# Linear attention, experts and a max MLP on one core: sums and floors moved to GpSimd, rows turned by transposes

## The chip, the core and the metric

The kernel runs on one core of a Trainium2 chip. A core has five engines with a queue each: TensorE (PE, matmuls into the PSUM banks; its weight loads are listed apart as PEld), VectorE (DVE), ScalarE (ACT), GpSimd (POOL) and SyncE (SP, which here only issues DMAs). They wait for each other through semaphores. The metric is the device time of one execution in microseconds, lower is better.

## The reference

```python
def _attn_ref(r, k, v, w, u):                     # B, H, S, D = 4, 8, 768, 48
    state = np.zeros((B, H, D, D))
    for t in range(S):
        cur = np.einsum('bhd,bhe->bhde', u[None] * kt, vt)
        y[:, :, t] = np.einsum('bhd,bhde->bhe', rt, state + cur)
        state = wt[:, :, :, None] * state + np.einsum('bhd,bhe->bhde', kt, vt)

def reference(...):
    x = attn_out.transpose(0, 2, 1, 3).reshape(3072, 384)
    x = _moe_ref(x, expert_emb, tau, w1, w2)      # one of 8 experts per token, by the largest
                                                  # dot with the unit embeddings, over tau
    h = max(x @ m1, x @ m2, x @ m3); return h @ w_out
```

What is computed in the part that the change touches: for each batch and head the gated linear attention, whose term r.(u*k) for a token's own key stands apart; the turning of its output into rows of tokens in DRAM; and for each token the dots with the 8 expert embeddings, their largest and the first expert that has it.

## The kernel before

**Stages.** Attention fills the first 176 us, the routing table lies between 176 and 198 us, and then the experts in slots of 432 tokens and the max MLP in blocks of 512 run on PE to the end. The change lies in the first stage alone.

**Pairs.** Attention goes over n = 0 to 15, a pair of heads of one batch each (four pairs to a batch, PAIRS = 4). The 768 positions of a pair are 6 chunks of 128 (CH); a half h is 3 chunks (HALF). The order on each engine is written out by hand as a loop over n, and only semaphores tie the engines together. For pair n+1, in the loop body of n:

- PE: rows_of(n-1, 0), keys(n) (turns the scaled keys to rows), turn_raw(n+1, "k"), scores(n, 1), turn_raw(n+2, "w"), rows_of(n-1, 1), turn_raw(n+1, "r"), key_values(n), mix_values(n) for both halves, mix_state(n), scores(n+1, 0). turn_raw turns the inputs from positions to columns by transposes, and the turn of w waits until VectorE has read the same banks for the keys.
- VectorE: mask(n, 0), own_of(n+1), keys_of(n+1), mask(n, 1), prefix_of(n+1), carry(n), receptance_of(n+1), suffix_of(n+2). suffix_of and prefix_of are the running products of the decay w, from behind and from the front, as scans of 774 elements (L948, L959). prefix_of first takes the floor of the chunks' products (L957) and its reciprocal (L958). own_of sums the products r*k*u of each position (L991). mask places the scores above the diagonal (L999).
- GpSimd: own_products(n+2) and own_times_u(n+2) make r*k and r*k*u in rku (L567, L572), and own_diagonal(n+1) spreads the own sums on a diagonal in score (L589), on which the mask of pair n+1 waits. Before own_products it waits for suffix_ok, before own_diagonal for prefix_ok, so each begins when a scan has ended.
- ScalarE: copies out of PSUM, among them x_cols (L695), x_rows (L703) and dot_parts (L705), and the stores of token rows to DRAM.

**Rows.** rows_of(n, h) multiplies the attention output x_cols (columns by positions) from the right by to_rows, 104 wide: an arranged identity of 96 columns that turns the pair into rows and puts its heads in order, and 8 columns of the expert embeddings, which give the pair's part of the dots. An fp32 matmul is two instructions in the trace, a transpose is one; so a half is x6.

**Batches.** When four pairs are done, add_dots(b) sums their four parts of the dots (L1021) and largest_of(b) finds the largest per token (L1028, L1029), in the body n = 4, 8 and 12, between carry and receptance; first_of(b) finds the first expert (L1035 to L1038) at the same place in n = 5, 9 and 13. The last batch follows behind the loop.

## Time and profile before

| | |
|---|---|
| median of 3 runs | 740.96 us (740.53 to 742.77) |
| profiled execution | 742.08 us, its span 740.3 |
| granted TensorE clock, mean | 0.98 |
| PE busy | 696.4 us, 94% of the span |
| VectorE busy | 415.2 us, 56% |
| ScalarE busy | 278.1 us, 38% |
| GpSimd busy | 129.3 us, 17% |

The profile is one execution. Shares over the span mix the stages: VectorE's share is 9 tenths or more in the slices up to about 150 us and falls behind them, while PE's is 9 tenths nearly throughout. In a timeline row the first number is the start, the second the time from the first start to the last end of what is merged there (x6: six instructions); a bracket tells how long the engine was idle before it and what ended that. Successive instructions of VectorE overlap by some 0.08 us, and a PE group's end is modelled, so the distance between starts tells more than the durations do.

### The profile page before, as it was taken

The page shows a single profiled execution, that of the slowest core. Times are in us where ns is not written, and L with a number is a line of the kernel's source. Part 1 is how long each engine was busy: PE and PEld are TensorE (multiplying, and loading weights), DVE is VectorE, ACT ScalarE, POOL GpSimd, SP SyncE. Part 2 cuts the span into 40 slices and gives each one's busy share as a digit, 9 for nine tenths or more (in the row PEclk, how much of TensorE's full clock was granted, in tenths as well). Part 3 has the DMA queues.
Part 4 walks back from the last instruction along what each step waited for, and adds up shares of the span by engine and source line. Part 5 has one row for each costly group of instructions (what it writes and reads, how often), then busy time and mean ns, then how long its engine had stood idle before and what let it go on. Part 6 is the DMA issues. An engine that isn't in the chain of part 4 may idle for free.

```text
span 740.3 us, 12783 instructions
## 1 busy us (share of the span) xinstructions
PE 696.4 (94%) x4794; PEld 626.3 (85%) x4794; DVE 415.2 (56%) x611; ACT 278.1 (38%) x584; POOL 129.3 (17%) x120
## 2 busy tenths in 40 slices
PE   6899999984799999999999999999999999999995
PEld 6788788873799999999999988888988988989875
DVE  7899999995766666554554545324233243242331
ACT  3355555555366665454444443112022021120110
POOL 4644444430522210000000000010100200201102
PEclk9999999998799999999999999999999999999998
DMA  9999998911475754433433400010000100100001
GB/s 147 171 193 190 143 161 144 221 34 34 144 230 168 212 170 128 130 119 93 127 107 105 127 21 1 1 43 1 22 22 1 43 0 1 43 1 21 23 0 43
DMA packets 148679, 66.44 MB, mean 90 GB/s; under 512 B 119560, under 2 KB 146320, under 8 KB 148624
## 3 DMA queue, kind: packets, MB, share of 16 engines
q1 hardware_dynamic: 131024, 51.13, 32.3%
q0 software_dynamic: 3072, 9.54, 4.1%
q10 hardware_dynamic: 14528, 5.03, 3.1%
q8 instruction: 35, 0.57, 0.3%
q14 instruction: 20, 0.16, 0.1%
HBM read 56.14 MB, written 9.54 MB: 89 GB/s over the span
## 4 chain that ended last, share of the span: by engine, by line
PE 85%; DVE 5%; issue 3%; SPq 2%; POOL 2%; DMA 1%; ACT 0%; DVEq 0%; POOLq 0%
PE bank L1375 13%; PE bank L1377 13%; PE bank L1376 13%; PE score_banks L1375 7%; PE score_banks L1377 7%; PE score_banks L1376 7%; PE turn_banks L1375 3%; PE turn_banks L1377 3%; PE turn_banks L1376 3%; PE bank L1493 3%; PE bank L1464 2%; PE score_banks L1422 2%; PE turn_banks L1409 2%; PE bank L1480 2%; DVE key_s L973 2%
## 5 line engine op out<-in xcount | busy, mean ns | idle before, releaser
L641 POOL DMA_INDIRECT out_dram<-o_put,slot_tok x24 | 25.2, 1052 | 438.8 <-DVE o_put L1345 438.8
L1375 PE MATMUL bank<-hh,w2h 128*128 128x432 f32 x192 | 69.0, 359 | 0.0
L1377 PE MATMUL bank<-hh,w2l 128*128 128x432 f32 x192 | 68.8, 358 | 0.0
L1376 PE MATMUL bank<-hl,w2h 128*128 128x432 f32 x192 | 68.8, 358 | 0.0
L1296 DVE SCALAR_TENSOR_TENSOR hl<-score_banks,hh 128x432 fp32r<-128x432 f32 x48 | 29.2, 608 | 66.6 <-ACT hh L841 65.7
L892 ACT CAST gh<-g 128x512 fp32r<-128x512 f32 x36 | 22.4, 621 | 106.7 <-PE bank L1377 60.7
L1375 PE MATMUL score_banks<-xh,w1h 128*128 128x432 f32 x144 | 53.6, 372 | 0.5 <-DVE xl L1256 0.5
L841 ACT ACTIVATE hh<-score_banks 128x432 fp32r<-128x432 f32 x48 | 25.5, 531 | 73.3 <-PE score_banks L1377 73.3
L1376 PE MATMUL score_banks<-xl,w1h 128*128 128x432 f32 x144 | 52.2, 363 | 0.0
L1377 PE MATMUL score_banks<-xh,w1l 128*128 128x432 f32 x144 | 52.2, 362 | 0.0
L1375 PE MATMUL bank<-moh,gh 128*128 128x384 f32 x144 | 48.8, 339 | 0.9 <-DVE gl L1363 0.9
L1354 DVE TENSOR_TENSOR g<-bank,g 128x512 f32<-128x512 f32 x18 | 12.5, 692 | 66.0 <-ACT g L888 66.0
L1376 PE MATMUL bank<-mol,gh 128*128 128x384 f32 x144 | 48.7, 338 | 0.0
L1377 PE MATMUL bank<-moh,gl 128*128 128x384 f32 x144 | 48.7, 338 | 0.0
L1345 DVE TENSOR_SCALAR o_put<-bank,slot_gate 128x384 f32<-128x384 f32 x24 | 14.8, 618 | 52.8 <-PE bank L1377 52.8
L1354 DVE TENSOR_TENSOR g<-turn_banks,g 128x512 f32<-128x512 f32 x18 | 12.5, 692 | 56.7 <-ACT g L888 56.7
L1375 PE MATMUL score_banks<-bh,mh 128*128 128x512 f32 x108 | 42.5, 394 | 0.0
L1375 PE MATMUL turn_banks<-bh,mh 128*128 128x512 f32 x108 | 42.5, 394 | 0.0
L1375 PE MATMUL bank<-bh,mh 128*128 128x512 f32 x108 | 42.5, 394 | 0.0
L1377 PE MATMUL turn_banks<-bh,ml 128*128 128x512 f32 x108 | 42.3, 392 | 0.0
L1377 PE MATMUL score_banks<-bh,ml 128*128 128x512 f32 x108 | 42.3, 392 | 0.0
L1377 PE MATMUL bank<-bh,ml 128*128 128x512 f32 x108 | 42.3, 392 | 0.0
(221 smaller groups left out, 1734.0 us busy)
## 6 DMA issues: line engine op xcount, KB each, us to landing
w_raw<-in_moe_w_dram SPq DMA_DIRECT2D x77, 384.0 KB, 3.3
raw_w<-in_w_dram SPq DMA_DIRECT2D x32, 144.0 KB, 3.9
raw_r<-in_r_dram SPq DMA_DIRECT2D x32, 144.0 KB, 4.6
vals<-in_v_dram SPq DMA_DIRECT2D x32, 144.0 KB, 3.6
x_tokens<-x_rows ACTq DMA_DIRECT2D x32, 144.0 KB, 3.5
raw_k<-in_k_dram SPq DMA_DIRECT2D x30, 144.0 KB, 4.4
w_raw<-in_moe_w_out_dram SPq DMA_DIRECT2D x3, 384.0 KB, 3.2
w_more<-in_moe_w_dram SPq DMA_DIRECT2D x2, 384.0 KB, 5.4
```

What stands on the lines that cost most here:

```text
L641: pool.indirect_dma_start(out=out, out_offset=bass.IndirectOffsetOnAxis(ap=slot_tok[:, n:n + 1], axis=0), in_=o_put[:, n % SB, :], in_offs ...
L841: act.activation(hh[:, f % UPS, :], bank[2 + f % 3][:, 0:SLOT], ACT.Relu).then_inc(hh_ok, 1)
L892: act.copy(gh[:, f, :], g2[:, :]).then_inc(gh_ok, 1)
L973: dve.tensor_tensor(key_s[:, n % 2].rearrange("q (x c) t -> q x c t", x=2), turned_half(turn_banks), products[:, n % 2, 0, :, 1:P + 1].rea ...
L1296: dve.scalar_tensor_tensor(out=hl[:, f % UPS, :], in0=bank[2 + f % 3][:, 0:SLOT], scalar=0.0, in1=f32(hh[:, f % UPS, :]), op0=ALU.max, op1 ...
L1354: dve.tensor_tensor(g1[:, :], bank[3 * (f % 2) + 1][:, :], g0[:, :], ALU.max).then_inc(g1_ok, 1)
L1375: pe.matmul(dst, sh, mh_, start=first, stop=False)
L1376: pe.matmul(dst, sh, ml_, start=False, stop=False)
L1377: return pe.matmul(dst, sl_, mh_, start=False, stop=last)
L1409: ins = pe.transpose(bank[x + (2 if name == "r" else 0)][:, j * P:(j + 1) * P], src, ident[:, :])
L1422: ins = pe.matmul(bank[2 + i][:, c * P:(c + 1) * P], key_s[rows, n % 2, HALF * h + c], rec_s[rows, n % 2, HALF * h + c], start=True, stop= ...
L1493: ins = pe.matmul(bank[7][:, c * (PW + E):(c + 1) * (PW + E)], x_cols[:, h, c], to_rows[:, h, p, :], start=True, stop=True)
```

## The change

Three things change in the attention stage.

- GpSimd gets more to do. own_times_u adds, after the multiplication by u, the upper 24 columns of each group of 48 in rku to the lower 24; VectorE's own_of reduces 24 columns. first_prefixes(n) takes the floor of the chunks' products into fore_floor; VectorE waits for it (fore_ok) and takes the reciprocal from there. dots_of(b) sums the four parts of a batch's dots in two steps, behind own_diagonal in the bodies n = 4, 8 and 12.
- On VectorE largest_of(b) stands behind receptance_of in n = 5, 9, 13 and first_of(b) behind it in n = 6, 10, 14.
- rows_of makes three transposes by the identity and then three matmuls of x_cols with emb_cols (8 columns). The heads' order, which to_rows gave for the second half, is now made by ScalarE's copy out of the bank (a negative step over the two 64-wide parts). The four copies that filled to_rows go.

```diff
             def own_times_u(n):
                 p = n % PAIRS
-                four = rku[:, n % 2].rearrange("q (c h) d -> q c h d", h=2)
-                pool.tensor_tensor(out=four, in0=four,
-                                   in1=u_row[...].broadcast_to([P, CH, 2, D]),
-                                   op=ALU.mult).then_inc(own_prod, 1)
+                both = rku[:, n % 2].rearrange("q (c h) d -> q c h d", h=2)
+                after(pool.tensor_tensor(out=both, in0=both,
+                                         in1=u_row[...].broadcast_to([P, CH, 2, D]),
+                                         op=ALU.mult))
+                pool.tensor_tensor(out=rku[:, n % 2, :, 0:D // 2], in0=rku[:, n % 2, :, 0:D // 2],
+                                   in1=rku[:, n % 2, :, D // 2:], op=ALU.add).then_inc(own_prod, 1)
...
+            def first_prefixes(n):
+                pool.wait_ge(suffix_ok, n + 1)
+                if n:
+                    pool.wait_ge(prefix_ok, n)
+                pool.tensor_scalar(fore_floor[:, :], products[:, n % 2, 0, :, 0], 1 / (LIMIT * 1e4), None, ALU.max
+                                   ).then_inc(fore_ok, 1)
...
+            def dots_of(b):
+                rows = slice(CH * b, CH * (b + 1))
+                pool.wait_ge(x_ready, 2 * PAIRS * (b + 1))
+                after(pool.tensor_tensor(out=two_parts[:, :, :, :], in0=dot_parts[:, rows, 0:2, :],
+                                         in1=dot_parts[:, rows, 2:4, :], op=ALU.add))
+                pool.tensor_tensor(out=dots[:, rows, :], in0=two_parts[:, :, 0, :], in1=two_parts[:, :, 1, :],
+                                   op=ALU.add).then_inc(dots_ok, 1)
...
+            first_prefixes(0)
             pool.wait_ge(prefix_ok, 1)
             own_products(0)
-            pool.wait_ge(suffix_ok, 2)
+            first_prefixes(1)
             own_times_u(0)
...
             for n in range(ALL - 1):
+                if n:
+                    first_prefixes(n + 1)
                 if n + 2 < ALL:
-                    pool.wait_ge(suffix_ok, n + 2)
                     own_products(n + 2)
                     own_times_u(n + 2)
                 pool.wait_ge(prefix_ok, n + 2)
                 own_diagonal(n + 1)
+                if n and n % PAIRS == 0:
+                    dots_of(n // PAIRS - 1)
...
             def prefix_of(n):
                 dve.wait_ge(suffix_ok, n + 1)
-                if n:
-                    dve.wait_ge(prefix_ok, n)
-                after(dve.tensor_scalar(fore_set[:, :, 0], products[:, n % 2, 0, :, 0], 1 / (LIMIT * 1e4), None, ALU.max))
-                after(dve.reciprocal(fore_set[:, :, 0], fore_set[:, :, 0]))
+                dve.wait_ge(fore_ok, n + 1)
+                after(dve.reciprocal(fore_set[:, :, 0], fore_floor[:, :]))
...
-                dve.tensor_reduce(out=own[...], in_=rku[:, n % 2], axis=AX, op=ALU.add)
+                dve.tensor_reduce(out=own[...], in_=rku[:, n % 2, :, 0:D // 2], axis=AX, op=ALU.add)
...
                 carry(n)
-                if n > 1 and n % PAIRS == 0:
-                    add_dots(n // PAIRS - 1)
-                    largest_of(n // PAIRS - 1, after)
-                if n > PAIRS and n % PAIRS == 1:
-                    first_of(n // PAIRS - 1, after)
                 if n + 1 < ALL:
                     receptance_of(n + 1)
-                else:
+                if n > PAIRS and n % PAIRS == 1:
+                    largest_of(n // PAIRS - 1, after)
+                if n > PAIRS and n % PAIRS == 2:
+                    first_of(n // PAIRS - 1, after)
+                if n + 1 == ALL:
                     judge()
...
                 for c in range(HALF):
-                    ins = pe.matmul(bank[7][:, c * (PW + E):(c + 1) * (PW + E)], x_cols[:, h, c],
-                                    to_rows[:, h, p, :], start=True, stop=True)
+                    pe.transpose(bank[7][:, c * P:(c + 1) * P], x_cols[:, h, c], ident[:, :])
+                for c in range(HALF):
+                    at = HALF * P + c * E
+                    ins = pe.matmul(bank[7][:, at:at + E], x_cols[:, h, c], emb_cols[:, h, p, :], start=True, stop=True)
```

PE's order before, for one pair: from scores(n, 1) (L1422) over the turn of w (L1409, into turn_banks), rows_of, the turn of r, key values (L1442), mix_values (L1464) and mix_state (L1480) to the next scores.

```order
L1422 MATMUL score_banks<-rec_s,key_s 128x128 x6
L1409 MATMUL turn_banks<-ident,raw_w 128x128 x6
L1493 MATMUL bank<-to_rows,x_cols 128x104 x3
L1409 MATMUL score_banks<-ident,raw_r 128x128 x6
L1442 MATMUL bank<-vals,key_rows 64x48 x10
L1464 MATMUL bank<-score,vals 64x128 x12
L1480 MATMUL bank<-rec_s,state 64x128 x10
L1422 MATMUL score_banks<-rec_s,key_s 128x128 x6
```

The same place after the change; the lines of before L1422, L1409, L1442, L1464 and L1480 are now L1440, L1427, L1460, L1482 and L1498.

```order
L1440 MATMUL score_banks<-rec_s,key_s 128x128 x6
L1427 MATMUL turn_banks<-ident,raw_w 128x128 x6
L1511 MATMUL bank<-ident,x_cols 128x128 x3
L1514 MATMUL bank<-emb_cols,x_cols 128x8 x3
L1427 MATMUL score_banks<-ident,raw_r 128x128 x6
L1460 MATMUL bank<-vals,key_rows 64x48 x10
L1482 MATMUL bank<-score,vals 64x128 x12
L1498 MATMUL bank<-rec_s,state 64x128 x10
L1440 MATMUL score_banks<-rec_s,key_s 128x128 x6
```

The order of the steps is the same; each rows_of is two groups in place of one, and here a matmul of the source counts as one.

VectorE before, at the batch steps of body n = 4: the prefix scan (L959), carry (L1006, L1015), the batch's sum and largest, receptance (L983), the suffix scan (L948).

```order
L959 SCALAR_TENSOR_TENSOR products<-decay,fore_set 128x774
L1006 SCALAR_TENSOR_TENSOR bank<-total,bank 128x240
L1015 TENSOR_TENSOR state<-bank,products 128x5x48
L1021 TENSOR_REDUCE dots<-dot_parts 128x48
L1028 TENSOR_REDUCE best<-dots 128x6
L1029 TENSOR_TENSOR maxed<-dots,best 128x48
L983 TENSOR_TENSOR rec_s<-score_banks,products 128x768
L948 SCALAR_TENSOR_TENSOR products<-decay,back_set 128x774
```

VectorE after, in body n = 5, from the second mask (L1018) on.

```order
L1018 COPY_PREDICATED score<-later,score_banks 128x2x3x128
L977 RECIPROCAL fore_set<-fore_floor 128x6
L978 SCALAR_TENSOR_TENSOR products<-decay,fore_set 128x774
L1025 SCALAR_TENSOR_TENSOR bank<-total,bank 128x240
L1034 TENSOR_TENSOR state<-bank,products 128x5x48
L1002 TENSOR_TENSOR rec_s<-score_banks,products 128x768
L1047 TENSOR_REDUCE best<-dots 128x6
L1048 TENSOR_TENSOR maxed<-dots,best 128x48
L969 SCALAR_TENSOR_TENSOR products<-decay,back_set 128x774
```

The sum is gone from VectorE, the largest stands behind receptance, and the floor ahead of the reciprocal is gone.

GpSimd after, in bodies n = 4 and 5: products, times u, half-add, diagonal, the batch's two sums, the next floor.

```order
L578 TENSOR_TENSOR rku<-raw_r,raw_k 128x576
L583 TENSOR_TENSOR rku<-rku,u_row 128x576
L586 TENSOR_TENSOR rku<-rku 128x12x24
L602 AFFINE_SELECT score<-own 128x1536
L611 TENSOR_TENSOR two_parts<-dot_parts 128x96
L613 TENSOR_TENSOR dots<-two_parts 128x48
L569 TENSOR_SCALAR fore_floor<-products 128x6
```

Before, only the first, second and fourth of these kinds stood here (L567, L572, L589).

## Rows read from the trace of the kernel before

**Rows 1.** Windows between starts of scores(n, 0): range, length, busy us (count) by engine, clock, DMA.
```profile
39.49:48.66 9.17, 8.84 (x124) 7.85 (x124) 9.05 (x12) 5.39 (x14) 4.39 (x3) 1.00 1.19 184
...
57.83:68.00 10.17, 8.85 (x125) 7.85 (x124) 9.94 (x15) 6.44 (x16) 4.38 (x3) 1.00 1.15 190
68.00:78.28 10.28, 8.86 (x124) 7.86 (x124) 10.09 (x15) 5.55 (x14) 4.39 (x3) 1.00 0.90 146
```

**Rows 2.** Timeline, VectorE, pair 3's period: start us, us, engine, line, op, shapes, [idle before].
```profile
51.09 0.74 DVE L991 TENSOR_REDUCE own<-rku 128x12 f32<-128x576 f32 x1
...
51.74 0.95 DVE L973 TENSOR_TENSOR key_s<-turn_banks,products 128x768 f32<-128x768 f32 x1
...
53.55 0.15 DVE L957 TENSOR_SCALAR fore_set<-products 128x6 f32<-128x6 f32 x1
...
53.96 1.77 DVE L959 TENSOR_TENSOR_SCAN products<-decay,fore_set 128x774 f32<-128x774 f32 x1
...
55.76 0.66 DVE L1006 TENSOR_TENSOR_SCAN bank<-total,bank 128x240 f32<-128x240 f32 x1
...
56.78 0.95 DVE L983 TENSOR_TENSOR rec_s<-score_banks,products 128x768 f32<-128x768 f32 x1
...
57.64 1.76 DVE L948 TENSOR_TENSOR_SCAN products<-decay,back_set 128x774 f32<-128x774 f32 x1
```

**Rows 3.** Timeline, PE, the same period and the next scores and rows.
```profile
50.82 0.82 PE L1409 MATMUL turn_banks<-ident,raw_k 128*128 128x128 f32 x6
...
52.84 0.85 PE L1409 MATMUL turn_banks<-ident,raw_w 128*128 128x128 f32 x6 [0.33 <-DVE key_s L973]
...
53.52 0.81 PE L1493 MATMUL bank<-to_rows,x_cols 128*128 128x104 f32 x6
...
54.17 0.82 PE L1409 MATMUL score_banks<-ident,raw_r 128*128 128x128 f32 x6
...
54.92 0.79 PE L1442 MATMUL bank<-vals,key_rows 128*64 128x48 f32 x20
...
57.83 0.94 PE L1422 MATMUL score_banks<-rec_s,key_s 64*128 64x128 f32 x12
...
58.70 0.92 PE L1493 MATMUL bank<-to_rows,x_cols 128*128 128x104 f32 x6
```

**Rows 4.** PE's weight loads: timeline of L1531; groups by line, mean ns behind the busy us.
```profile
173.90 0.30 PEld L1531 LDWEIGHTS turn_banks<-bad,all_ones 128*128 128x128 f32 x2
...
L1493 PEld LDWEIGHTS bank<-to_rows,x_cols 128*128 128x128 f32 x144 | 17.9, 191 | 1.4
...
L1409 PEld LDWEIGHTS turn_banks<-ident,raw_k 128*128 128x128 f32 x72 | 8.2, 141 | 0.0
```

**Rows 5.** Timeline, batch steps: VectorE's sum and first-expert product, GpSimd's select beside it.
```profile
65.95 0.48 DVE L1021 TENSOR_REDUCE dots<-dot_parts 128x48 f32<-128x192 f32 x1
...
76.12 0.64 DVE L1035 TENSOR_TENSOR maxed<-maxed,expert_no 128x48 f32<-128x48 f32 x1
...
75.16 1.55 POOL L589 TENSOR_SCALAR_AFFINE_SELECT score<-own 128x1536 f32<-128x1536 f32 x1 [2.58 <-DVE products L959]
```

**Rows 6.** Timeline, pairs 0 to 2: GpSimd, then VectorE.
```profile
24.72 1.75 POOL L567 TENSOR_TENSOR rku<-raw_r,raw_k 128x576 f32<-128x576 f32 x1 [2.50 <-DMA raw_r<-in_r_dram]
26.54 1.41 POOL L572 TENSOR_TENSOR rku<-rku,u_row 128x576 f32<-128x576 f32 x1
...
22.25 0.75 DVE L991 TENSOR_REDUCE own<-rku 128x12 f32<-128x576 f32 x1 [1.41 <-POOL rku L572]
...
27.02 2.55 DVE L948 TENSOR_TENSOR_SCAN products<-decay,back_set 128x774 f32<-128x774 f32 x1
31.02 1.01 DVE L999 COPY_PREDICATED score<-later,score_banks 128x768 f32<-128x768 int32 x1 [1.45 <-POOL score L589]
```

**Rows 7.** Timeline, ScalarE: the copy of the turned embeddings.
```profile
8.65 0.44 ACT L733 COPY to_rows<-bank 48x64 f32<-48x64 f32 x2 [0.78 <-PE bank L1392]
```

**Rows 8.** Timeline, PE: the key values of pair 15.
```profile
169.93 0.79 PE L1442 MATMUL bank<-vals,key_rows 128*64 128x48 f32 x20 [1.01 <-issue]
```

More of the change, by code:

```diff
@@ L133, in linear_attention_moe_max_mlp @@
     x_rows = sb("x_rows", [P, XR, HALF, PW])
-    to_rows = sb("to_rows", [P, 2, PAIRS, PW + E])
+    emb_cols = sb("emb_cols", [P, 2, PAIRS, E])
     squares = sb("squares", [E, DM])
@@ L701, in tokens_of @@
                     act.wait_ge(x_stored[s % XR], 16 * (s // XR))
-                src = bank[7][:, 0:HALF * (PW + E)].rearrange("q (c e) -> q c e", c=HALF)
-                act.copy(x_rows[:, s % XR], src[:, :, 0:PW]).then_inc(rows_out, 1)
+                src = bank[7][:, 0:HALF * P].rearrange("q (c i d) -> q c i d", c=HALF, i=2)[:, :, ::1 - 2 * h, 0:D]
+                act.copy(x_rows[:, s % XR].rearrange("q c (i d) -> q c i d", i=2), src).then_inc(rows_out, 1)
                 first = CH * b + HALF * h
-                act.copy(dot_parts[:, first:first + HALF, p, :], src[:, :, PW:]).then_inc(x_ready, 1)
+                act.copy(dot_parts[:, first:first + HALF, p, :],
+                         bank[7][:, HALF * P:HALF * (P + E)].rearrange("q (c e) -> q c e", c=HALF)).then_inc(x_ready, 1)
                 act.wait_ge(rows_out, s + 1)
@@ L724, in _ @@
             act.wait_ge(rows_clear, 1)
-            for x in range(2):
-                for i in range(2):
-                    rows = slice(64 * (i ^ x), 64 * (i ^ x) + D)
-                    act.copy(to_rows[rows, x, :, D * i:D * (i + 1)],
-                             ident[rows, rows].unsqueeze(1).broadcast_to([D, PAIRS, D])).then_inc(emb_ready, 1)
             act.wait_ge(emb_turned, 1)
@@ L732, in _ @@
                 rows = slice(64 * i, 64 * i + D)
-                act.copy(to_rows[rows, :, :, PW:], bank[7][rows, 0:2 * PAIRS * E].rearrange(
+                act.copy(emb_cols[rows, :, :, :], bank[7][rows, 0:2 * PAIRS * E].rearrange(
                     "q (x p e) -> q x p e", x=2, p=PAIRS)).then_inc(emb_ready, 1)
@@ L990, in own_of @@
                     dve.wait_ge(own_ready, n - 1)
-                dve.tensor_reduce(out=own[:, n % 2].rearrange("q c h -> q (c h)"), in_=rku[:, n % 2], axis=AX, op=ALU.add
+                dve.tensor_reduce(out=own[:, n % 2].rearrange("q c h -> q (c h)"), in_=rku[:, n % 2, :, 0:D // 2], axis=AX, op=ALU.add
                                   ).then_inc(own_sum, 1)
```

11 lines of the change are left out of this document (7 added, 4 removed).

## Prediction, made before the changed kernel was run

> **What bounds the kernel now.** I read the page's busy shares first: PE 94% of the span. But every edit lies in the first 176 us, the attention stage, so I cut that stage at the starts of scores(n, 0), the PE step that opens the work on head pair n. From 39.49 us on, the distance is 9.17 us; in six of the next twelve it is 10.17 or 10.28 [rows 1]. In 9.17 us VectorE is busy 9.05 and PE 8.84: two engines sit at the limit together.
>
> The chain of waits says the same of one period. VectorE's starts follow each other without a gap: own sum 51.09, keys 51.74, floor 53.55, prefix scan 53.96, carry 55.76, receptance 56.78, suffix scan 57.64 [rows 2]. PE looks as if it had 0.33 us of air, its wait for keys at 52.84, but that wait is a detour of its own path: the turn of k ends at 50.82 + 0.82 = 51.64, VectorE's keys runs from 51.74 to 52.69 and the turn of w follows at 52.84; of these 1.2 us PE can fill 0.87 with scores(n, 1), as long as scores(n, 0) takes from 57.83 to 58.70 [rows 2, 3]. From the key values at 54.92 the route through carry (55.76), state and receptance (56.78 + 0.95 = 57.73) reaches scores at 57.83, and PE's own steps end there too [rows 2, 3]. So what is added on PE anywhere in a period lengthens it; what is taken from VectorE alone does not shorten it. **The six long periods are VectorE's**: batch sums and largest values in one, the first-expert step in the next, 1.00 and 1.11 us more; PE waits in them.
>
> **What the change takes from VectorE.** Per period the floor goes: its 0.15 us and the handover to the reciprocal, 0.18. The own sum reduces 24 instead of 48 columns per group; from 0.74 us for 576 elements I put 288 at 0.45, 0.29 less (0 to 0.37). Three batch sums of 0.48 go [rows 5]. The largest and the first steps stay but stand behind receptance, off PE's path, half a us or so each. VectorE's work per period falls to 8.7, and to 9.2 or 9.35 where a batch step stands. Three times two long periods therefore lose what made them long: 3 x 2.11 = 6.3 us, the whole gain. The rest of VectorE's saving is idle time, because PE is at 9.17.
>
> **What it adds to PE.** A half of rows_of was 3 fp32 matmuls, 6 in the trace, each with its own 128-column load; the half at 53.52 ends at 54.17, 0.108 us for each [rows 3]. It becomes 3 transposes and 3 matmuls with 8 moving columns, in the trace 3 + 6 = 9. What does one of 8 columns cost? The nearest row has a single moving column: the 128x1 matmul of L1531. Its two weight loads together take 0.30 us and one such load takes 0.19, so the second began 0.11 after the first [rows 4]: the load sets the pace, however few columns move. By plain count a half gains 3 x 0.107 = 0.32 us. Two things take some off: a transpose's load is 0.05 shorter than a matmul's (141 against 191 ns) [rows 4], which shows at the first load of the half at 58.70, and the last matmul streams 8 columns, not 104, ahead of the next group (0.04). I take +0.24 for the half at 58.70 and +0.28 for that at 53.52, +0.52 a period (bounds 0.45 to 0.64). As receptance and keys have slack now, 0.02 may come back: 9.67 us.
>
> The Trainium skill has a rule that would make the new form cheap: the page "TensorE: Matmul & The Clock Gate", section Back-to-back issue gap, gives 1 to 64 moving columns an issue floor of about 25 ns. By it the six small matmuls are an estimated 0.15 us, and the half would get shorter. L1531's loads speak against it; the rule is given for a matmul alone.
>
> Twelve periods from 39.49: before 6 x 9.17 + 3 x 10.17 + 3 x 10.28 = 116.4; after 12 x 9.67 = 116.0, plus what follows.
>
> **What it adds to GpSimd.** Per pair: a floor on 6 columns, which I put at 0.2 (0.1 to 0.4; VectorE took 0.15), and a half-add of 288 elements. The multiplication by u takes 1.41 for 576 [rows 6]; 0.8 for the half (0.7, in proportion, to 1.41, no saving). In the loop GpSimd has room, it is busy 4.39 of 9.17 us [rows 1], but not at any moment: a VectorE scan and a GpSimd instruction exclude each other. The suffix scan at 27.02 took 2.55 us instead of 1.76 because GpSimd's product at 26.54 ran until 27.95 [rows 6], and the small product on VectorE at 76.12 took 0.64, until the select begun at 75.16 had ended [rows 5]. The Trainium skill, page "GPSIMD Engine Reference", the table's line on SBUF interfaces, names this contention for VectorE instructions with two SBUF inputs or in a 2-port mode; both rows fit it, and whether the reciprocal is held no row here shows.
>
> Counted from scores(n, 0): the suffix scan ends near 1.6, floor 1.7, products 1.9 to 3.3, times u to 4.8, half-add 4.85 to 5.65. The prefix scan wants to begin at 5.3, so it waits 0.3 and ends at 7.4. Carry must wait for the key values until 7.5: the stall is covered by 0.1 us. In the two periods behind a largest or a first step GpSimd's chain is 0.5 to 0.7 later, the half-add begins just when the scan wants to and lies wholly in front of it or between, and carry comes 0.2 to 0.4 late. That is 0.6 a batch, for two batches 1.2 us (0 to 2.5); the third falls on pair 14, where PE turns no w and has air. The batch sums on GpSimd (about 0.7) lie before the suffix scan and cost 0.1.
>
> **What moves at no cost.** ScalarE's four copies into to_rows go; the next thing it does, the copy of the turned embeddings, waited 0.78 us for PE behind them anyway [rows 7]. Its copy out of the rows bank reads the same 288 elements in another order. SP's store of a batch's dots waits for GpSimd instead of VectorE, a period later at most; SP has by then no load to issue that a pair waits for behind it, since the stores stand behind all raw loads. VectorE's reciprocal waits for GpSimd's floor, 3 us old by then. If GpSimd were late, keys and masks would not be queued behind that wait, but the prefix scan and carry would.
>
> **The first two pairs.** Here VectorE waits for GpSimd: 1.41 us at the own sum of 22.25, 1.45 at the mask of 31.02 [rows 6]. Two half-adds and a floor with their gaps delay the own sum to about 24.3. The prefix scan behind it now meets the products of pair 2, which start at 24.72 in both kernels since they wait for raw_r, and comes 2.7 us or more late. Some of it is absorbed by the old waits at 31.02 and by loads that have come meanwhile. Followed on to scores(2, 0) it leaves 39.49 + 1.4 us (0 to 3).
>
> **The end.** Pair 14: +0.2. Pair 15 has three halves in line: one ahead of ScalarE's copies on which the key values of 169.93 wait [rows 8], then its own two: +0.8.
>
> **Sum**, against the profiled run's 742.08 us (span 740.3 and 1.8 around it): start +1.4, twelve periods -0.4, collisions +1.2, pair 14 +0.2, end +0.8 gives +3.2; I round down to +3.0 for the front of pair 2, where much waits on loads. Behind 176 us nothing changes. The median of the runs shown, 740.96, is 1.1 below the profiled run; the same difference gives 744.0.
>
> **Rivals.**
> (a) The small matmuls' loads hide behind their neighbours and only columns count: 8 of 104 columns' 0.108 is 0.01 each, with some issue up to 0.025. A half is then 3 x 0.108 + 6 x 0.01 to 0.025 = 0.38 to 0.47, about 0.23 shorter, and PE's period 8.7. The Trainium skill's issue floor above points the same way. Now VectorE sets it: 8.7 and a scan held 0.5 behind GpSimd, 9.2, and 0.48 or 0.67 more in the batch steps' periods, of which I let 2.9 us show in all. 12 x 9.2 + 2.9 = 113.3 against 116.4, start +1.4, end -0.7: -2.4, or 738.6, faster; with GpSimd's adds at their low bound 736. For it: nothing but the columns; against it: [rows 4]. It decides from about 0.075 us for a small matmul down: a half then costs 3 x 0.108 + 6 x 0.075 = 0.77, 0.12 more than now, 2 x 0.12 x 12 + 0.4 = 3.3 in all, and the 6.3 us won at the batch steps outweigh that, the start and the collisions together.
> (b) GpSimd's half-add is 1.2 us or more, or the floor 0.4: the prefix scan ends past 7.5 in every period, and 0.25 x 12 + 1.5 in the start and the collisions are added: 748.5. For it: only 0.1 us covers it.
> (c) The old rows pace was partly slack and half of the 0.52 is absorbed: 12 x 0.26 = 3.1 less, 740.9, no change. For it: PE's 0.33 wait; against it: that wait is a round trip of PE's own.
>
> **Chances.** Forecast 0.60, at 744.0 (own range 742 to 746.5, from the bounds 0.45 to 0.64 and those of the collisions); (a) 0.15, half of it below 738.7; (b) 0.13; (c) 0.12. About 0.3%, 2.2 us, is what a measurement of this kernel can tell from no change: below 738.7 faster, above 743.2 slower. The forecast case has 0.17 of its 0.60 below 743.2. Slower 0.43 + 0.13 = 0.56; same 0.17 + 0.12 + 0.07 = 0.36; faster 0.08. The range for 8 in 10: 739.5 to 748.0, which leaves out the low end of (a) and the top of (b).
>
> **What would show it.** Right: periods near 9.7, none at 10.2 but two or four near 9.9 to 10; PE's rows half 0.9 us or more with loads 0.11 apart; VectorE idle about 0.6 a period; the prefix scan at 2.0 us rather than 1.77; scores(2, 0) near 40.9. Wrong: loads of the small matmuls closer than 0.075 apart; periods below 9.4; a prefix scan that isn't lengthened. A clock below 1.0 between 40 and 170 us would upset all of it.

## Result and profile after the change

| | before | after |
|---|---|---|
| median of 5 runs each | 740.96 us (739.6 to 742.94) | 746.71 us (744.27 to 747.55) |
| ratio | | 1.0052, 95% interval 1.0029 to 1.0075 |
| profiled execution, its span | 742.08, 740.3 us | 746.71, 744.9 us |
| granted TensorE clock, mean | 0.98 | 0.976 |
| PE busy | 696.4 us | 707.0 us |
| VectorE busy | 415.2 us | 406.2 us |
| GpSimd busy | 129.3 us | 153.2 us |

The kernel became slower by 0.3 to 0.75%. VectorE lost 9 us of work, PE gained 10.6 and GpSimd 24. The difference of the two profiled spans, 4.6 us, lies in these stretches:

| stretch | before | after | difference |
|---|---|---|---|
| to scores(2, 0) | 39.49 | 41.92 | +2.43 |
| the twelve periods from there to scores(14, 0) | 116.37 | 117.04 | +0.67 |
| pair 14 | 9.03 | 9.05 | +0.02 |
| scores(15, 0) to the last batch sum | 11.37 | 11.98 | +0.61 |
| from that sum to the end | 564.1 | 564.9 | +0.8 |

The last line is mostly scatter. Nothing is changed there, and in the eleven other profiles of this study with the same work behind the sum it lies between 562.2 and 564.7 us.

Windows of after between starts of scores(n, 0) (range, length, then busy us and count of PE, weight loads, VectorE, ScalarE and GpSimd, granted clock, DMA share, GB/s):

```profile
41.92:51.65 9.73, 9.40 (x131) 8.40 (x130) 8.76 (x11) 5.46 (x14) 5.37 (x5) 1.00 0.73 154
61.38:71.11 9.73, 9.40 (x132) 8.41 (x130) 8.77 (x11) 5.45 (x14) 6.02 (x7) 1.00 0.74 154
90.56:100.44 9.88, 9.46 (x131) 8.39 (x130) 9.12 (x14) 5.44 (x14) 6.78 (x5) 1.00 0.72 151
```

Against [rows 1]: every period is 9.73 us, with the batch sums in it (second line) or without; only the two behind a first-expert step are 9.88. PE's work rose from 8.84 to 9.40 us, the same 0.56 by which the period rose. VectorE's fell from 9.05 to 8.76 and bought nothing.

Timeline of after, PE, in the period from 61.38 (start us, us, engine, line, op, shapes, [idle before and what ended it]), to be laid beside [rows 3]:

```profile
62.25 0.55 PE L1511 MATMUL bank<-ident,x_cols 128*128 128x128 f32 x3
62.63 0.73 PE L1514 MATMUL bank<-emb_cols,x_cols 128*128 128x8 f32 x6
63.22 0.74 PE L1450 MATMUL bank<-ident,key_s 128*128 128x128 f32 x5
63.80 0.82 PE L1427 MATMUL turn_banks<-ident,raw_k 128*128 128x128 f32 x6
...
65.82 0.84 PE L1427 MATMUL turn_banks<-ident,raw_w 128*128 128x128 f32 x6 [0.33 <-DVE key_s L992]
66.50 0.49 PE L1511 MATMUL bank<-ident,x_cols 128*128 128x128 f32 x3
66.83 0.73 PE L1514 MATMUL bank<-emb_cols,x_cols 128*128 128x8 f32 x6
67.42 0.85 PE L1427 MATMUL score_banks<-ident,raw_r 128*128 128x128 f32 x6
68.20 0.79 PE L1460 MATMUL bank<-vals,key_rows 128*64 128x48 f32 x20
68.82 1.50 PE L1482 MATMUL bank<-score,vals 128*64 128x128 f32 x24
```

The second half of rows runs from 66.50 to 67.42: 0.92 us for 3 turns and 6 instructions of 8 columns, where the old one took 0.65 from 53.52 to 54.17. The six small ones alone take 0.59, 0.10 each. The first half takes 0.97. PE's wait for the keys is 0.33 as before.

VectorE and GpSimd in the same period, beside [rows 2]:

```profile
63.77 0.43 DVE L1010 TENSOR_REDUCE own<-rku 128x12 f32<-128x288 f32 x1
64.71 0.96 DVE L992 TENSOR_TENSOR key_s<-turn_banks,products 128x768 f32<-128x768 f32 x1 [0.51 <-issue]
...
66.72 1.93 DVE L978 TENSOR_TENSOR_SCAN products<-decay,fore_set 128x774 f32<-128x774 f32 x1
69.03 0.66 DVE L1025 TENSOR_TENSOR_SCAN bank<-total,bank 128x240 f32<-128x240 f32 x1 [0.39 <-PE bank L1460]
```

```profile
63.04 0.23 POOL L569 TENSOR_SCALAR fore_floor<-products 128x6 f32<-128x6 f32 x1 [2.50 <-DVE products L969]
63.23 1.42 POOL L578 TENSOR_TENSOR rku<-raw_r,raw_k 128x576 f32<-128x576 f32 x1
64.73 1.41 POOL L583 TENSOR_TENSOR rku<-rku,u_row 128x576 f32<-128x576 f32 x1
66.22 0.80 POOL L586 TENSOR_TENSOR rku<-rku 128x288 f32<-128x288 f32 x1
```

The half-add ends at 67.02, and the prefix scan begun at 66.72 takes 1.93 instead of 1.77: the scan is held until the half-add is done. It does no harm here, since carry then waits 0.39 us for PE. VectorE's idle time is 0.9 us a period.

### The profile page after: what moved, and what is told of

Read it like the earlier page. It is cut to its first block, busy times and chain, and to the rows that moved or that the text cites. A ratio compares the mean times of both kernels' runs of the same rounds, so it can differ in the third digit from the quotient of the medians.

```text
span 744.9 us, 12991 instructions
## 1 busy us (share of the span) xinstructions
PE 707.0 (95%) x4890; PEld 636.2 (85%) x4890; DVE 406.2 (55%) x592; ACT 277.4 (37%) x580; POOL 153.2 (21%) x158
## 3 DMA queue, kind: packets, MB, share of 16 engines
q0 software_dynamic: 3072, 9.54, 4.0%
HBM read 56.14 MB, written 9.54 MB: 88 GB/s over the span
## 4 chain that ended last, share of the span: by engine, by line
PE 88%; DVE 5%; issue 3%; POOL 2%; DMA 1%; ACT 0%; ACTq 0%; DVEq 0%; POOLq 0%
PE bank L1393 13%; PE bank L1395 13%; PE bank L1394 13%; PE score_banks L1393 7%; PE score_banks L1395 7%; PE score_banks L1394 7%; PE turn_banks L1393 3%; PE turn_banks L1395 3%; PE turn_banks L1394 3%; PE bank L1482 3%; PE bank L1514 2%; PE score_banks L1440 2%; PE turn_banks L1427 2%; PE bank L1511 2%; PE bank L1498 2%
```

## The experiments

"Period" is the distance between starts of scores(n, 0) without batch steps; b1 and b2 are the two long ones behind a batch. "Pair 1" and "pair 2" are the starts of their scores.

| kernel | median us | ratio, interval | pair 1 | pair 2 | period | b1, b2 | last sum |
|---|---|---|---|---|---|---|---|
| before | 740.96 | | 28.13 | 39.49 | 9.17 | 10.17, 10.28 | 176.25 |
| after | 746.71 | 1.0052, 1.0029 to 1.0075 | 29.38 | 41.92 | 9.73 | 9.73, 9.88 | 179.99 |
| e1 rows alone | 748.35 | 1.0103, 1.0077 to 1.0129 | 27.34 | 39.19 | 9.73 | 10.72, 10.53 | 182.58 |
| e2 all but rows | 738.82 | 0.9955, 0.9937 to 0.9974 | 29.64 | 40.42 | 9.23 | 9.37, 9.58 | 172.75 |
| e3 batch steps alone | 737.10 | 0.9941, 0.9919 to 0.9962 | 28.24 | 38.55 | 9.17 | 9.66, 9.88 | 171.85 |
| e4 after, clock kept up | 742.73 | 1.0009, 0.9994 to 1.0023 | 29.89 | 39.62 | 9.73 | 9.73, 9.88 | 177.69 |
| e5 e3 + floor | 737.03 | 0.9926, 0.9908 to 0.9944 | 27.82 | 36.99 | 9.17 | 9.66, 9.88 | 170.23 |
| e6 e3 + half-add | 741.69 | 0.9986, 0.9974 to 0.9998 | 29.58 | 40.35 | 9.47 | 9.57, 9.79 | 175.63 |
| e7 e5, clock kept up | 736.38 | 0.9910, 0.9892 to 0.9928 | 28.54 | 37.71 | 9.17 | 9.66, 9.88 | 170.93 |
| e9 before again | 743.03 | 1.0003, 0.9985 to 1.0021 | 28.20 | 40.44 | 9.17 | 10.17, 10.27 | 177.22 |
| e10 e6, half-add later | 741.72 | 0.9981, 0.9970 to 0.9993 | 30.20 | 39.74 | 9.35 | 9.89, 10.10 | 175.30 |
| e11 e5, steps spread | 736.19 | 0.9907, 0.9891 to 0.9922 | 27.92 | 37.09 | 9.17 | 9.37 to 9.53 | 169.55 |
| e12 e11, clock kept up | 734.88 | 0.9891, 0.9875 to 0.9906 | 28.20 | 37.37 | 9.17 | 9.36 to 9.52 | 169.83 |

### The three parts of the change

**e1** is the kernel before with the new rows alone:

```diff
-                    ins = pe.matmul(bank[7][:, c * (PW + E):(c + 1) * (PW + E)], x_cols[:, h, c],
-                                    to_rows[:, h, p, :], start=True, stop=True)
+                    pe.transpose(bank[7][:, c * P:(c + 1) * P], x_cols[:, h, c], ident[:, :])
+                for c in range(HALF):
+                    at = HALF * P + c * E
+                    ins = pe.matmul(bank[7][:, at:at + E], x_cols[:, h, c], emb_cols[:, h, p, :], start=True, stop=True)
```

> The kernel before with nothing changed but the turning of rows (three transposes and three 8-column matmuls, ScalarE's reordering copy). Theory (PE's weight loads are added to every period): the normal period is 9.73 us as in the changed kernel, not 9.17, while the six batch-step periods stay VectorE's at 10.2 and 10.3, so 6 x 0.56 = 3.4 us in the twelve periods and 0.6 at the end, +4 us, ratio 1.005 to 1.006. Rival (PE had slack, the collisions with GpSimd made the changed kernel slower): normal period 9.2 to 9.4, +1 us or less.

Its windows:

```profile
39.19:48.92 9.73, 9.40 (x131) 8.41 (x131) 9.11 (x12) 5.41 (x14) 4.38 (x3) 1.00 1.19 184
58.65:69.37 10.72, 9.40 (x130) 8.39 (x131) 10.02 (x15) 6.45 (x16) 4.38 (x3) 1.00 1.07 171
```

The period is that of after to the hundredth, so the new rows alone set it: +0.56. The long periods were a miss, and with them the ratio: the last sum is 6.3 us later than before, not 4. PE's new work did not vanish in VectorE's long periods, it was added to them: in full in the first of a batch (10.72), by 0.25 in the second (10.53), where the first-expert product now takes 0.34 instead of 0.64 [rows 5], as GpSimd's select beside it is nearer to its end. The batch steps stood between carry and receptance, where PE waits, and the rows stand where VectorE waits. Both are pieces of one path, and their prices add up.

**e2** is the change with the old rows (the same lines turned back, with to_rows and its copies).

> The changed kernel with the old turning of rows: all that moved to GpSimd, and the batch steps behind receptance. Theory: PE's 9.17 us is the floor of the period, VectorE needs 8.7 and is held about 0.4 by the half-add, so normal periods are 9.2 to 9.3 and batch-step periods at most 9.8: twelve periods 112.5 instead of 116.4, -3 to -4 us with a start that costs up to 1, ratio 0.995. Rival (GpSimd's adds are what made the changed kernel slower): periods of 9.7 remain and the ratio is 1.000 to 1.005.

Without the rows the rest of the change is a gain of 0.3 to 0.6%, with the periods that were expected. **e3** takes from that rest the batch steps alone: the sums on GpSimd, largest and first behind receptance.

```diff
+                if n and n % PAIRS == 0:
+                    dots_of(n // PAIRS - 1)
...
-                if n > 1 and n % PAIRS == 0:
-                    add_dots(n // PAIRS - 1)
-                    largest_of(n // PAIRS - 1, after)
-                if n > PAIRS and n % PAIRS == 1:
-                    first_of(n // PAIRS - 1, after)
                 if n + 1 < ALL:
                     receptance_of(n + 1)
...
+                if n > PAIRS and n % PAIRS == 1:
+                    largest_of(n // PAIRS - 1, after)
+                if n > PAIRS and n % PAIRS == 2:
+                    first_of(n // PAIRS - 1, after)
```

> The kernel before with only the batch's sum of dots on GpSimd and largest and first steps behind receptance one period later; floor, own sum and rows as before. Theory (the whole gain lies in the batch steps): normal periods stay 9.17, batch-step periods fall from 10.17 and 10.28 to about 9.66 and 9.85, for VectorE still has to do them, 3 x 0.95 = -2.8 us, some of it lost to the sum on GpSimd that lies beside the suffix scan (up to 3 x 0.5). -1.5 to -2.8 us, ratio 0.997. Rival (PE's path hides them wholly once they are behind receptance): -6 us.

The batch steps alone bring as much as all of e2, whose interval overlaps. The periods came as expected, the gain was larger: 4.4 us at the last sum instead of at most 2.8. The first two batches give 1.8, the third, whose steps fall mostly behind the twelve periods, 1.7, and pair 2 is 0.9 earlier, of which the last section tells. **e5** adds the floor on GpSimd, **e6** in its place the half-add, with the floor left on VectorE:

```diff
+                pool.tensor_tensor(out=rku[:, n % 2, :, 0:D // 2], in0=rku[:, n % 2, :, 0:D // 2],
+                                   in1=rku[:, n % 2, :, D // 2:], op=ALU.add).then_inc(own_prod, 1)
...
-                dve.tensor_reduce(out=own[:, n % 2].rearrange("q c h -> q (c h)"), in_=rku[:, n % 2], axis=AX, op=ALU.add
+                dve.tensor_reduce(out=own[:, n % 2].rearrange("q c h -> q (c h)"), in_=rku[:, n % 2, :, 0:D // 2], axis=AX, op=ALU.add
```

> The batch-steps-only kernel plus the floor on GpSimd; own sum and rows as before. Theory (normal periods are PE's 9.17, batch-step periods VectorE's sum): VectorE is 0.18 shorter, so normal periods stay 9.17, and the two long periods of a batch fall from 9.66 and 9.88 to about 9.5 and 9.7; -0.9 us against the batch-steps-only kernel, ratio 0.993. Rival (the floor's 0.23 us on GpSimd pushes products and times u into the prefix scan): periods 9.3 and no gain, ratio 0.995 or more.

> The batch-steps-only kernel plus the half-add on GpSimd and the shorter own sum; floor and rows as before. Theory (the half-add is what holds the prefix scan and lengthens the first pairs): VectorE is 0.3 shorter but is held about as long, so normal periods are 9.17 to 9.25, batch-step periods about 9.4 to 9.6, and scores(2, 0) comes 1 to 2 us later than in the batch-steps-only kernel: ratio 0.995, worse than batch steps alone by 0.5 to 1.5 us. Rival (the floor is what costs, the half-add is a gain): ratio below 0.993.

The floor's move costs nothing (e5 and e3 overlap), but it did not shorten the long periods as expected: they stay at 9.66 and 9.88, and e11 below shows why. The half-add takes back 0.45%: period 9.47, where 9.17 to 9.25 was expected, pair 1 at 29.58. Timeline of e6, VectorE:

```profile
52.22 0.44 DVE L1005 TENSOR_REDUCE own<-rku 128x12 f32<-128x288 f32 x1
52.90 0.96 DVE L987 TENSOR_TENSOR key_s<-turn_banks,products 128x768 f32<-128x768 f32 x1 [0.24 <-issue]
...
54.68 0.61 DVE L971 TENSOR_SCALAR fore_set<-products 128x6 f32<-128x6 f32 x1
55.33 0.19 DVE L972 RECIPROCAL fore_set<-fore_set 128x6 f32<-128x6 f32 x1
55.55 1.77 DVE L973 TENSOR_TENSOR_SCAN products<-decay,fore_set 128x774 f32<-128x774 f32 x1
```

And GpSimd beside it:

```profile
54.47 0.80 POOL L577 TENSOR_TENSOR rku<-rku 128x288 f32<-128x288 f32 x1
```

The half-add runs from 54.47 to 55.27. VectorE's floor of 6 elements, 0.15 us alone, begins at 54.68 and ends when the half-add does. The 0.3 us that the shorter own sum saves turn into a wait of 0.24 ahead of the keys (the view has it as issue; PE's turn of k ends just before), while the 0.45 lost behind them lie on the path, and 0.30 of it reaches the period.

In e2 the floor is on GpSimd, and the half-add of the same length holds the scan itself. VectorE, then GpSimd:

```profile
54.75 2.18 DVE L982 TENSOR_TENSOR_SCAN products<-decay,fore_set 128x774 f32<-128x774 f32 x1
```

```profile
54.51 0.79 POOL L586 TENSOR_TENSOR rku<-rku 128x288 f32<-128x288 f32 x1
```

The scan is 0.41 longer, but it began 0.22 earlier, as the floor isn't in front of it: period 9.23. So the floor's move is worth something only where the half-add has come as well.

**e10** is e6 with one more GpSimd instruction of 6 elements ahead of each pair's products, which puts the half-add later:

```diff
+                pool.tensor_scalar(delay_out[:, :], products[:, n % 2, 0, :, 0], 1 / (LIMIT * 1e4), None, ALU.max
+                                   ).then_inc(delayed, 1)
```

> The version with the half-add on GpSimd and the floor on VectorE (741.69 us, periods of 9.47 to 9.55 us), with one more GpSimd instruction of 6 elements ahead of the products of each pair, whose output nobody reads. It puts the half-add about 0.25 us later. My theory, that the half-add hurts there because it starts just ahead of VectorE's floor and holds it and the prefix scan behind: now floor and scan come first, the half-add is the one that waits, and the period falls to 9.2 to 9.35 us, the time to about 738.5 us, ratio 0.996. Rival, that the half-add costs by its length wherever it lies, or that GpSimd's chain is itself the late one: the period stays at 9.5 us or grows to 9.7 us, and the ratio is 0.999 to 1.002.

VectorE, then GpSimd:

```profile
53.96 0.15 DVE L982 TENSOR_SCALAR fore_set<-products 128x6 f32<-128x6 f32 x1
54.14 0.20 DVE L983 RECIPROCAL fore_set<-fore_set 128x6 f32<-128x6 f32 x1
54.37 2.10 DVE L984 TENSOR_TENSOR_SCAN products<-decay,fore_set 128x774 f32<-128x774 f32 x1
```

```profile
54.05 0.80 POOL L586 TENSOR_TENSOR rku<-rku 128x288 f32<-128x288 f32 x1
```

Half a hit. The half-add now begins 0.09 behind the floor's start, the floor takes 0.15 again and the period falls by 0.12, though the half-add still comes ahead of the scan and holds it for 0.3. That more GpSimd work makes the period shorter rules out the rival for the normal periods. The time did not follow: it is that of e6, not 738.5, for b1 and b2 grew by 0.3 each. In them the multiplication by u, made later by the extra instruction, reaches into VectorE's floor. GpSimd, then VectorE, in b1:

```profile
81.19 1.42 POOL L583 TENSOR_TENSOR rku<-rku,u_row 128x576 f32<-128x576 f32 x1
```

```profile
82.24 0.40 DVE L982 TENSOR_SCALAR fore_set<-products 128x6 f32<-128x6 f32 x1
```

In e6 the same floor takes 0.16, and the scan behind it 2.13; here the floor takes 0.40 and the scan 2.21. In these periods the rival's second half is right: GpSimd's chain is the late one.

### What a small matmul costs

**e8** is the change with one small matmul a half instead of three, 24 columns wide; it leaves out the dots of two chunks of three, so that tokens go to other experts and the part behind 176 us differs (761.33 us, not to be compared). Only the periods count.

```diff
-                for c in range(HALF):
-                    at = HALF * P + c * E
-                    ins = pe.matmul(bank[7][:, at:at + E], x_cols[:, h, c], emb_cols[:, h, p, :], start=True, stop=True)
+                ins = pe.matmul(bank[7][:, HALF * P:HALF * (P + E)], x_cols[:, h, 0],
+                                emb_cols[:, h, p, :].unsqueeze(1).broadcast_to([P, HALF, E]), start=True, stop=True)
```

> The changed kernel with one small matmul per half in place of three: it multiplies the first chunk by the embeddings three times over (24 moving columns), so the dots of two chunks in three are left out; four of the six small instructions go, the moving columns stay 24. Theory (each small instruction costs its 128-column load, 0.107 us): a half is 0.43 shorter, PE's period would be 8.87, and the period becomes what VectorE and GpSimd give in the kernel with the old rows, 9.2 to 9.3, batch-step periods 9.4 to 9.6; ratio 0.995 to 0.997. Rival (columns or the change between forms set the price): periods stay at 9.6 to 9.73 and the ratio at 1.005.

```profile
71.68 0.49 PE L1511 MATMUL bank<-ident,x_cols 128*128 128x128 f32 x3
72.00 0.30 PE L1512 MATMUL bank<-emb_cols,x_cols 128*128 128x24 f32 x2
72.15 0.85 PE L1427 MATMUL score_banks<-ident,raw_r 128*128 128x128 f32 x6
```

The half takes 0.47 instead of 0.92: four instructions less are 0.45 less, 0.11 each, with the same 24 columns in all. Instructions are paid here, each with its 128-column load, and columns are not. An instruction without such a load does not cost that much: the key values above, 20 instructions of 48 columns with loads of 64, run from 68.20 to 68.82, 0.03 each. Few columns behind a shorter load were not tried. The periods are 9.21 to 9.25 us, 9.44 behind a first-expert step: this is the world of rival (a), which had put them at 9.2. The expectation of the ratio was missed, for the reason above.

Behind each batch sum e8 has a period of 8.82 us. VectorE's scan in the period before it, and in it:

```profile
62.66 2.38 DVE L978 TENSOR_TENSOR_SCAN products<-decay,fore_set 128x774 f32<-128x774 f32 x1
71.90 1.77 DVE L978 TENSOR_TENSOR_SCAN products<-decay,fore_set 128x774 f32<-128x774 f32 x1
```

GpSimd's half-add in the same two:

```profile
62.62 0.80 POOL L586 TENSOR_TENSOR rku<-rku 128x288 f32<-128x288 f32 x1
71.93 2.33 POOL L586 TENSOR_TENSOR rku<-rku 128x288 f32<-128x288 f32 x1
```

In the first the half-add begins 0.04 ahead of the scan and holds it. In the second the scan gets in 0.03 ahead, and now the half-add is the one that waits (2.33 us) and nobody waits for it. A shift of 0.07 us between the two engines is the difference between 9.24 and 8.82, in all three batches. This shows what e10 aimed at; and 8.82 is PE's own period, for which 8.87 was expected.

### The start and the clock

**e4** is the change with 36 and 42 small bf16 matmuls on PE in the waits of pair 0, written to a bank that is not in use:

```diff
             def mix_state(n):
+                if n == 0:
+                    warm(42)
                 pe.wait_ge(state_ready, n + 1)
...
                 scores(n, 1)
+                if n == 0:
+                    warm(36)
```

> The changed kernel with 36 and 42 small bf16 matmuls on PE (without use) where PE waits in pair 0, ahead of the turn of w for pair 2 and ahead of the state product. Theory (the start's extra time is PE at half clock from 29 to 36 us behind its waits): granted clock stays 1.0 from 25 to 37 us, scores(1, 1) and the steps around it go at full pace, and scores(2, 0) starts at 39.5 instead of 41.9: 2.4 us less than the changed kernel, ratio to before 1.002 to 1.003. Rival (GpSimd's longer chain delays the start): scores(2, 0) stays at 41 to 42 and the ratio at 1.005.

A window of after, then of e4:

```profile
30.00:35.00 5.00, 5.00 (x30) 4.67 (x27) 2.37 (x3) 1.73 (x6) 3.62 (x4) 0.50 1.09 218
```

```profile
30.00:35.00 5.00, 4.67 (x50) 4.22 (x51) 4.67 (x5) 2.29 (x8) 3.13 (x5) 1.00 0.94 189
```

In after PE waits 2.57 us for VectorE's state at 25.9 to 28.47, and from 29.5 to 36.3 it runs at a granted clock of 0.50, the lower of the two levels: the turn of k takes 1.42 us to the next start instead of 0.75. Pair 1's period is 12.54 there and 9.73 in e4, though e4 was 0.51 later at pair 1. The clock is 2.8 us of the start in this profile; at the last sum e4 is 2.3 ahead, and its ratio is back at 1.

The wait alone does not bring this on. e8 and e10, which have no extra matmuls, wait 2.44 and 2.15 us at the same place and stay at 1.00 from there to 45 us, with 8.86 and 9.54 us for pair 1's period; e2 and e6 wait 3.7 us and have 0.50 for some 3.3 us, with 10.8. So how much of the 2.8 comes with the change and how much with the one execution stays open. A part of it is there in each run: the mean granted clock is 0.974 to 0.979 in the five of after and 0.978 to 0.987 in the twelve of e4.

**e7** puts 24 and 30 of them into e5.

> The batch-and-floor kernel with 24 and 30 small bf16 matmuls without use where PE waits in pair 0. Theory (a low-clock stretch in the first 40 us costs what a gap on PE brings on): granted clock 1.0 from 20 to 37 us and scores(2, 0) 1 us or more earlier than without them, about 37.5; ratio 0.991. Rival (the start waits for GpSimd and loads, whatever the clock): scores(2, 0) within 0.3 us of the batch-and-floor kernel's.

It settles nothing: e5 had the full clock from 20 us on without them, and pair 2 is no earlier (37.71 against 36.99).

**e9** is the kernel before, once more.

> The kernel before, unchanged, profiled and timed once more, to see how much of the start is the execution's own and not the kernel's. My theory: ratio 1.000 within 0.003; the periods behind pair 2 are 9.17 us again, those with batch steps 10.1 to 10.3 us, and the scores of pair 2 begin within 1 us of 39.5 us. Rival, that the 2.4 us by which the change was late at pair 2 are scatter of the first loads' landing: the scores of pair 2 begin here more than 1.5 us away from 39.5 us.

Pair 2 is at 40.44, 0.95 later than in the first profile, and the ratio is 1 within its interval. The first loads are not the reason. At pair 1 the two profiles are 0.07 apart and at pair 2's turn of w 0.19 (33.68 and 33.87); then e9 has a granted clock of 0.50 from 34.6 to 38.0, where the first profile has 1.00 throughout:

```profile
35.00:40.00 5.00, 5.00 (x71) 4.50 (x72) 4.18 (x6) 2.41 (x5) 2.14 (x2) 0.70 1.30 191
```

So the kernel before has such stretches too, in some executions, and of the +2.43 at pair 2 some 1 us may be the execution's own. Pair 1 is steadier. In the six profiles with a half-add (after, e2, e4, e6, e8, e10) it lies at 29.4 to 30.4, in the eight without one at 27.3 to 28.5: 29.9 on average against 28.1, so the half-add costs some 1.8 us there, whatever else is changed; e6 and e3, which differ by it and the shorter own sum alone, are 1.3 apart.

### The best version

**e11** is e5 with the five remaining VectorE steps of a batch in five pairs, one in each (the last batch of the loop: three in pair 15); **e12** has the extra matmuls too.

```diff
-                if n > PAIRS and n % PAIRS == 1:
-                    largest_of(n // PAIRS - 1, after)
-                if n > PAIRS and n % PAIRS == 2:
-                    first_of(n // PAIRS - 1, after)
+                for b in range(B - 1):
+                    for i, at in enumerate((0, 1, 2, 3, 4) if b < B - 2 else (0, 1, 2, 2, 2)):
+                        if n == PAIRS * (b + 1) + 1 + at:
+                            batch_step(b, i, after)
```

> The version with the batch steps moved behind the receptance and the floor on GpSimd (737.03 us, ratio 0.9926), with the five remaining steps on VectorE spread over five pairs, one a pair, where there they stood two in one pair and three in the next. My theory, that a pair has some 0.4 to 0.5 us of room on VectorE behind the receptance and the longer periods (9.66 and 9.88 us) are what goes beyond it: with one step of 0.27 to 0.65 us a pair the periods are 9.17 to 9.35 us, the gain is 2 to 3 us more, ratio 0.989 to 0.990. Rival, that GpSimd's sums of the dots, which hold VectorE off, make the long periods and not the steps: then one period a batch stays at 9.6 us or more, and the ratio is 0.992 to 0.993.

> The same with the 24 and 30 extra small matmuls in the first pair's waits of TensorE. My theory: the granted clock is 1.00 from 20 to 40 us, the scores of pair 2 begin at 37 to 38 us, and the time is 0 to 1 us below that of the version without them, ratio 0.988 to 0.990. Rival, that the extra matmuls only replace waits where the clock was full anyway: no difference within 0.3%.

The periods are 9.37 where a step stands, and 9.48 or 9.53 once a batch. None stays at 9.6, so GpSimd's sums aren't what makes them long; but my theory was as wrong. There is no room behind receptance at all. e5, VectorE, and the first scores that follow on PE:

```profile
82.33 0.95 DVE L1004 TENSOR_TENSOR rec_s<-score_banks,products 128x768 f32<-128x768 f32 x1
83.20 0.20 DVE L1056 TENSOR_TENSOR maxed<-maxed,expert_no 128x48 f32<-128x48 f32 x1
83.43 0.20 DVE L1058 TENSOR_REDUCE lead<-maxed 128x6 f32<-128x48 f32 x1
83.67 0.21 DVE L1059 TENSOR_TENSOR hot<-lead,expert_no 128x48 bf16<-128x48 f32 x1
83.95 1.77 DVE L971 TENSOR_TENSOR_SCAN products<-decay,back_set 128x774 f32<-128x774 f32 x1
```

```profile
86.69 0.94 PE L1442 MATMUL score_banks<-rec_s,key_s 64*128 64x128 f32 x12 [0.33 <-DVE score L1020]
88.28 0.85 PE L1429 MATMUL turn_banks<-ident,raw_w 128*128 128x128 f32 x6 [0.65 <-DVE key_s L994]
```

Three steps put the suffix scan 0.7 us later, the first mask and the keys with it, and PE waits 0.33 and then 0.65 for them: the period is 9.17 + 0.71. Two steps give 9.66, one 9.37. While PE's period is 9.17, each 0.2 us step behind receptance costs 0.2 or more, in whichever pair it stands. Spreading them gained 0.7 us at the last sum, not 2 to 3. In e12 the clock is 1.00 from 20 us on, where e11 has a mean of 0.71 from 20 to 25, but pair 2 is no earlier (37.37 against 37.09) and the last sum neither. Its ratio lies where it was expected without the reason for it, and its interval overlaps e11's; 0.8 to 1.25% below the kernel before is the best of the study.

## Why the prediction held, step by step

**The bound** was read rightly, on the main point: PE's added work lengthened every period, and what VectorE lost did not shorten the normal ones. VectorE's work was put at 8.7 and is 8.76; the terms that are named for it give 8.6 (9.05 less 0.15 and 0.29), and the rest is the scan's 0.16 of waiting for the half-add.

**The small matmuls** were priced by their loads [rows 4], at 0.107; e8 gives 0.11. The page "TensorE: Matmul & The Clock Gate" of the Trainium skill (section Back-to-back issue gap) has a floor by which it would be an estimated 25 ns, but gives it for the matmul alone and says that in a stream of loads and matmuls both set the spacing. The runs agree with the second: 0.10 in after and 0.11 in e8, with a 128-column load each. The period came out at 9.73, not 9.67: the two halves cost +0.22 and +0.27 (taken: 0.24 and 0.28), but the group behind each took 0.03 to 0.04 longer to its next start, where I had put 0.04 to the credit, and the 0.02 given back never came. Over twelve periods that is +0.7.

**The batch steps** gave the predicted gain, but one reason was wrong. I had them "off PE's path" behind receptance. e5 and e11 show that they are on it at a PE period of 9.17; in after they are hidden only because the rows made PE's period 0.56 longer. What really went is the sum (0.48), and GpSimd's hold on the first-expert product, 0.64 before [rows 5] and 0.20 in its new place. In e3 that is 0.51 and 0.40 per batch within the loop, and the whole 2.1 for the third batch, whose steps fall on pairs 14 and 15 and cost 0.45 there (9.48 against 9.03).

**The collisions** were put at 1.2 us and cost 0.3 (twice 0.15). I had the carry covered by 0.1 us only; it has 0.39, since the key values on PE come later as well. That this and the period's error cancel is luck: 116.0 + 1.2 forecast, 117.04 measured.

**The start** was put at +1.4 (0 to 3) and measured +2.43; that it lies in the range is luck too, for two terms were missed, of opposite sign. The products of pair 2, which I had waiting for raw_r until 24.72 in both kernels [rows 6], began at 22.90: the loads had become faster, of which the last section tells. The own sum of pair 1 came at 22.98, not 24.3. Pair 1 is 1.25 late. In its period PE's clock, which had no term, costs up to 2.8 (e4); without that the period is 1.6 shorter than before (9.73 in e4 against 11.36), where the mask had waited 1.45 us for a GpSimd chain that began late for want of raw_r [rows 6]. **The end** was +0.61 instead of +0.8, **pair 14** +0.02 instead of +0.2.

**The sum** was +3.0; the ratio gives +3.9 us (2.1 to 5.6), the medians +5.7, the profiles +4.6 with 0.8 of scatter in it. The median of 746.71 is 2.7 above the forecast of 744.0 and just outside its own range, which ended at 746.5; part of that is the kernel before, whose median was 740.96 in these five runs and 742.7 to 743.0 in the 17 to 23 runs beside each group of experiments. Of the terms, the start was the one most mis-sized. The half-add took 0.80 and the floor 0.23, as taken, so rival (b) did not come; nor did (c), as e1's full 0.56 shows.

## What to carry to other kernels

- An fp32 matmul of few columns with a stationary tile of its own costs its load. Folding 8 columns into a matmul that loads the same tile anyway was cheaper than splitting them off, though the rest could then be a plain transpose.
- When two engines are tied, work taken from one is worth nothing, and work added to either was paid in full here, even at a place that looks off the path, but for e1's second long period. Ask of each move what waits behind it within the period, not only what waits for it.
- GpSimd's work beside VectorE is free only where it does not start just ahead of a VectorE instruction that it holds, such as a scan; in e8 0.07 us in their order made 0.4 us a period.

## What the runs showed of the hardware

**VectorE and GpSimd shut each other out, for some of VectorE's instructions.** With GpSimd at work, a VectorE floor of 6 elements took 0.61 instead of 0.15 us, a scan 2.18 instead of 1.77 and once 2.89 (after, at 24.53); held by the scan, the half-add took 2.33 instead of 0.80. Whoever starts first finishes first. The scans of 774 elements, the floors and the first-expert product are held so. The masks, the own sum, the keys, the carry, the state, the receptance and the reciprocal are not: in the attention stage of all fourteen profiles they take the same within 0.06 us with GpSimd at work as without, as the keys at 64.71 beside the multiplication by u at 64.73, 0.96 us.

**The loads land in a third less time in every kernel that has two_parts.** I had not expected it, and no line of the diff speaks of it. Loads from 5 to 26 us of e9 (the kernel before) and e11, of one chip:

```profile
DMA packets 18198, 3.44 MB, mean 164 GB/s; under 512 B 18197, under 2 KB 18197, under 8 KB 18197
...
raw_r<-in_r_dram SPq DMA_DIRECT2D x4, 144.0 KB, 4.5
```

```profile
DMA packets 23588, 4.45 MB, mean 212 GB/s; under 512 B 23587, under 2 KB 23587, under 8 KB 23587
...
raw_r<-in_r_dram SPq DMA_DIRECT2D x6, 144.0 KB, 3.0
```

A load of 144 KB lands after 3.0 instead of 4.5 us. Before, e9 and e1 have the slower loads, the other eleven the faster ones, chip by chip (e1, e2, e3 and e4 ran on one, e9 to e12 on another). The same shows in the loop: a DMA share of 1.19 for 184 GB/s in before [rows 1] and e1, of 0.73 for 154 GB/s in after. What the eleven have in common is the tile two_parts, 384 bytes a partition, laid out ahead of the raw tiles and pushing them up. By the sizes in the kernel raw_w begins at 27552 in the three and at 27936 in the eleven (27968 in e10). The loads are rows of 192 bytes at every 256; from 27552, which is 160 above a multiple of 256, each row crosses such a multiple, and from 27936 or 27968, 32 or 64 above, none does. That fits all fourteen profiles, but it was not tried alone, and is not shown: a run of the kernel before with its tiles moved by 384 bytes is missing. So it stays open how much of the start's gain in e3, e5, e11 and e12 (pair 2 at 38.55 to 36.99 against 39.49 and 40.44) belongs to the batch steps' edit and how much to the layout that came with it; the shorter periods don't depend on it, since e1 and after have the same one at either speed.
